# Scores of two steps in one bank, and z of the last tiles in halves, in a fused attention and expert kernel

## The chip, the cores and the metric
The kernel runs on one core of one Trainium2 chip. The metric is the device time of one execution in microseconds (us); lower is better. All times in this document are of that core. TensorE (PE) multiplies, VectorE (DVE), ScalarE (ACT) and GpSimd (POOL) work on its results, and SyncE (SP) issues the transfers. PSUM, into which PE writes, has eight banks of 512 fp32 columns on 128 partitions.

## The reference
For each of 4 batch entries ("rows" in the kernel) of 576 tokens:
```
scores = q k^T / 8 + bias(head) ; causal, window of 128 ; softmax ; @ v    (8 heads of 64)       stage 1
h = relu(x @ w_in) ; u, v = halves ; v = layernorm(v)
y = (u * (w_spatial @ v + b)) @ w_out                                                             stage 2
logits = y @ w_gate ; the two best of 4 experts, weights by softmax over the two
each expert e: q,k,v = y @ wq[e],wk[e],wv[e] (64 wide); full causal softmax(q k^T / 8) @ v @ wo[e]
out = sum over the chosen experts of weight * that                                                stage 3
```
All of it is in fp32 accuracy. Large products are made of three products of rounded parts (high by high, high by low, low by high), so almost every operand exists as a "high" part (ScalarE copies it out of PSUM) and a "low" part (VectorE subtracts the high part from the same PSUM bank).

## The kernel before
The order of the work on each engine is written out by hand, once per engine, and the engines meet at counting semaphores. The 576 tokens are five tiles, four of 128 and one of 64.

**Stage 1** of a row goes in 10 steps `m`, two steps to a tile of queries. A step holds two groups, `g = 2m` and `2m + 1`, of two heads each. The path of a group: PE `scores1(m)` (both groups of a step, L1199) writes banks 0 and 1; DVE `bias1(g)` (L833) adds the bias, writes the scores to a ring in SBUF and keeps the row minimum; ACT `exp1(g)` (L576); DVE `reciprocal1(g)` (L842, L844); POOL multiplies, `scale1(g)` (L471); PE `transpose1(g)` (L1242) into bank 2 or 3; ACT `copy_pt1(m)` (L617) copies the even group out and DVE `copy_pt1_second(m)` (L900) the odd one; PE `values1(g)` (L1280) multiplies by v. Every step's scores use the same two banks, so `scores1(m)` waits on `s1_bi` until the biases of step m - 1 have been added. `scores1` runs two steps ahead of the transposes (`AHEAD1 = 2`). In the first tile a head's scores are 128 columns wide, in the next three tiles 256, in the last 192. Step by step PE also does a piece of the product x @ w_in (`v_product`), from step 2 on (step 3 in row 0).

**Stage 3** first makes q and k of the experts in eight products `qk_product(0..7)` (L1212 to L1214). `high_qk(i)` on ACT (L709, L712) and `low_qk(i)` on DVE (L1103, L1108) take them out of PSUM. The products 4 to 7 reuse banks 2 and 3 in turn, so `qk_product(i)` waits until `low_qk(i - 2)` is done. Between them lie the scores of the first tiles (`scores3(w)`, L1429 and L1435, 18 units `w`). DVE also works out the weights of the experts, in two parts, `top2_a` and `top2_b` (`top2_b(0)` is L1042 to L1058, eight small operations one after the other). Then the loop of 8 steps: in a step PE does `transpose3` of two groups (L1447), the scores of two later units, an `out_product(b, i)` when z of tile i is ready (L1212 to L1214, L1218 and L1219 for the short tile), and `values3` of two groups (L1467). DVE `max3` (L1012), ACT `exp3` (L735), DVE `reciprocal3` (L1077, L1079), POOL `scale3` (L554), and the copies `copy_pt3` (ACT, L744) and `copy_pt3_second` (DVE, L1068) lie between. The tiles come in the order 0, 1, 4, 2, 3; tile i of this order ends in step 0, 1, 3, 5, 7. `values3` adds z transposed in bank 6 or 7 (by the parity of i); after a tile's last step `high_z(i)` (ACT, L749) and `low_z(i)` (DVE, L1084) take it out; `out_product` writes into the same bank; `copy_out(b, i)` (ACT, L608; for the short tile L604 and then `add_out`, DVE, L1091) takes the result out for the store.

**The seam.** While stage 3 of row b ends, stage 1 of row b + 1 begins: PE issues `scores1(b + 1, 0..2)` in the steps 5, 6 and 7, DVE and ACT interleave `bias1`, `exp1` and `reciprocal1` of the first groups, and `out_product(b, 4)` of the last tile comes in step 0 of the next row, behind its first two transposes. There are three such seams; the last row has none and ends with `out_product(3, 4)`, its copy and its store.

Of the kernel before, what the change touches and what calls it, by code (L numbers as in the profile page):

```python
# [27 lines left out]
P = 128  # L28
# [95 lines left out]
def build(nc, qT, kT, v, w_in, wsT, bsp, woT, wcat, wo, out):  # L124
    ctx = ExitStack()
    with ctx:
# [191 lines left out]
        def s1_banks(b, m):  # L318
            return (6, 7) if b == 0 and m == 1 else S1_BANKS

# [248 lines left out]
        def _(act):  # L569
# [40 lines left out]
            def row(b, first, more):  # L610
# [42 lines left out]
                for m in range(ND1):  # L653
                    if m % 2 == 0 and m >= 2:
                        high_x(m // 2 - 1)
                    if m == 0 and not first:
                        copy_pt1(0)
                        exp1(b, 3)
# [91 lines left out]

                if first:
# [69 lines left out]
        def _(dve):  # L821
            def bias1(b, g):
# [3 lines left out]
                at = w * (g % 2)  # L826
                dve.wait_ge(s1_sc, ND1 * b + g // 2 + 1)
                for n, (u, h) in enumerate(units1(g)):
                    if qb < NT - 1:
                        scores, table = bank[:, s1_banks(b, g // 2)[n], at:at + w], bias[:, h, c0:c0 + w]  # L830
                    else:
                        scores, table = bank[:, S1_BANKS[g % 2], 0:w], bias_last[:, h // 2, :]
# [60 lines left out]
            def row(b, first, more):  # L893
# [36 lines left out]
                for m in range(ND1):  # L930
                    if m % 2 == 0 and m >= 2:
                        low_x(m // 2 - 1)
                    if m == 1 or (m == 0 and not first):
                        copy_pt1_second(m)
                    if 2 * m + 4 < NG1:
# [3 lines left out]
                    if m > 1 or (m == 0 and first):  # L939
                        copy_pt1_second(m)  # L940
                    if 2 * m + 5 < NG1:
# [138 lines left out]

                def low_z(i):
                    dve.wait_ge(s3_zh, NT * b + i + 1)
# [57 lines left out]
                for m in range(ND3):  # L1140
                    for i in range(NT - 1):
                        if m == DEND3[i] + 1:
                            low_z(i)
                    if m and len(units3(m - 1)):
# [10 lines left out]
                    if m == DEND3[ORDER3.index(NT - 1)] + 2:  # L1155
                        add_out(ORDER3.index(NT - 1))
# [3 lines left out]
                    if more and m == ND3 - 3:  # L1160
                        bias1(b + 1, 0)
                        bias1(b + 1, 1)
                    if more and m == ND3 - 2:
# [16 lines left out]
        def _(pe):  # L1180
            def scores1(b, m):
# [7 lines left out]
                if m:  # L1189
                    if b or m != 1:  # L1190
                        pe.wait_ge(s1_bi, U1 * b + units1(2 * m if b or m > 2 else 2 * m - 2)[0][0])
                for j in range(2):
# [3 lines left out]
                    for odd in range(2):  # L1196
                        half = slice(D * odd, D * odd + D)
                        to = bank[:, s1_banks(b, m)[odd], w * j:w * j + w] if qb < NT - 1 else bank[half, S1_BANKS[j], 0:w]
# [46 lines left out]
            def out_product(b, i):  # L1245
                r = rows(ORDER3[i])
                pe.wait_ge(s3_zl, NT * b + i + 1)
                if i == 0 and b == 0:
                    pe.wait_ge(s_wlo, 2 * KT + NT + 2)
                for k in range(2):  # L1250
# [6 lines left out]
                last.then_inc(s3_om, 1)  # L1257
# [3 lines left out]
            def row(b, first, more):  # L1261
# [60 lines left out]
                for m in range(ND1):  # L1322
                    if (2 <= m or (m == 0 and first)) and m + AHEAD1 < ND1:
                        scores1(b, m + AHEAD1)
                    transpose1(b, 2 * m)
# [3 lines left out]
                    if m == 1:  # L1329
# [121 lines left out]
                def values3(g):  # L1451
# [6 lines left out]
                    elif es[0] == 0 and i >= 2:  # L1458
                        pe.wait_ge(s3_o, NT * b + i - 1)
                    if g % 2:  # L1460
# [3 lines left out]
                    for kb in ks:  # L1464
                        for j, e in enumerate(es):
                            c, at = place(qb, ks, len(es), j, kb), r * (e // 2)
                            last = nc.tensor.matmul(bank[D * (e % 2):D * (e % 2) + D, 6 + i % 2, at:at + r],  # L1467
# [27 lines left out]
                for m in range(ND3):  # L1495
# [8 lines left out]
                    for i in range(NT - 1):  # L1504
# [44 lines left out]
```

## Time and profile before
| | |
|---|---|
| median of 3 runs | 513.32 us (513.13 to 514.11) |
| the profiled execution | 514.02 us, span 512.2 us |
| PE busy | 493.8 us, 96% of the span |
| DVE, ACT, POOL busy | 300.5, 275.9, 201.3 us |
| TensorE clock granted | full in every slice |

The span is the time from the first to the last instruction. Busy time is summed over an engine's instructions; the chain of waits is followed back from the last instruction of the kernel to whatever released each step. A wait's idle time is counted from the modelled end of the matmul before it.

### The profile page before, as it was taken

Reading aid. Unit: us, or ns where it says so; the run is one execution under the profiler, and the core shown is the slowest. Engines: PE = TensorE matmul, PEld = TensorE weight load, DVE = VectorE, ACT = ScalarE, POOL = GpSimd, SP = SyncE. Lnnn points to the kernel's source line nnn. Section 1 sums busy time; section 2 is a strip of 40 time slices with the busy share of each in tenths; the row PEclk is TensorE's granted clock in tenths of the full one; section 3 lists DMA queues with packets and bytes.
Section 4 is the critical chain, followed back from the end, with each engine's and each line's share of the span. In section 5 each row is a group of like instructions: output and inputs, shape, how many; then the busy total and the mean of one; then the engine's idle time right before and its main releaser. Section 6 shows DMA issues by size and latency. Waiting matters only on the chain.

```text
span 512.2 us, 10892 instructions
## 1 busy us (share of the span) xinstructions
PE 493.8 (96%) x3981; PEld 426.5 (83%) x3981; DVE 300.5 (59%) x1116; ACT 275.9 (54%) x820; POOL 201.3 (39%) x376
## 2 busy tenths in 40 slices
PE   8899999999999999999998999999998999999996
PEld 5677998998767789999876789999876779999974
DVE  6976772567757743256757762237676664236671
ACT  6876472446567643255657743236557663234572
POOL 4765432212424633423424553341244455162240
PEclk9999999999999999999999999999999999999999
DMA  8909020023110070004110061002311000000111
GB/s 245 320 25 287 24 82 1 1 47 96 49 43 1 4 184 1 1 1 127 54 32 22 2 158 29 1 1 47 114 34 41 1 3 1 1 0 16 33 43 52
DMA packets 31785, 28.51 MB, mean 56 GB/s; under 512 B 5810, under 2 KB 24242, under 8 KB 31732
## 3 DMA queue, kind: packets, MB, share of 16 engines
q1 hardware_dynamic: 31732, 27.82, 18.4%
q8 instruction: 31, 0.51, 0.4%
q14 instruction: 22, 0.18, 0.1%
HBM read 20.74 MB, written 4.72 MB: 50 GB/s over the span
## 4 chain that ended last, share of the span: by engine, by line
PE 78%; DVE 12%; ACT 4%; issue 3%; POOL 1%; DVEq 0%; ACTq 0%
PE bank L1212 15%; PE bank L1213 14%; PE bank L1214 14%; PE bank L1199 7%; PE bank L1242 5%; PE bank L1280 5%; PE bank L1429 5%; PE bank L1467 4%; PE bank L1447 4%; DVE ring L833 2%; DVE neg L1012 2%; PE bank L1219 1%; PE bank L1218 1%; PE bank L1370 1%; PE bank L1372 1%
## 5 line engine op out<-in xcount | busy, mean ns | idle before, releaser
L471 POOL TENSOR_SCALAR ring<-ring,r 128x256 f32<-128x256 f32 (+2 forms) x144 | 68.2, 486 | 88.1 <-DVE r L844 87.8
L554 POOL TENSOR_SCALAR p<-p,r,wgt 128x128 f32<-128x128 f32 (+3 forms) x64 | 38.4, 613 | 91.3 <-DVE r L1079 64.5
L576 ACT ACTIVATE ring<-ring,neg 128x256 f32<-128x256 f32 (+2 forms) x144 | 67.8, 473 | 6.7 <-DVE neg L833 6.6
L735 ACT ACTIVATE p<-bank,neg 128x128 f32<-128x128 f32 (+4 forms) x72 | 39.1, 548 | 41.2 <-DVE neg L1012 41.1
L833 DVE CUSTOM_DVE_ANT_0 ring<-bank,bias 128x256 f32<-128x256 f32 (+1 forms) x128 | 43.8, 384 | 14.9 <-PE bank L1199 14.9
L1199 PE MATMUL bank<-k,q 64*128 64x256 f32 (+2 forms) x320 | 40.7, 375 | 4.4 <-DVE neg L833 4.4
L519 POOL TENSOR_TENSOR g_lo<-uT,g_hi 128x288 fp32r<-128x288 f32 x32 | 27.2, 873 | 42.6 <-ACT g_hi L697 42.6
L1280 PEld LDWEIGHTS bank<-pt,v_in 128*64 128x64 f32 x576 | 28.2, 136 | 14.8 <-issue 11.6
L1212 PE MATMUL bank<-g_hi,w_c_hi 128*128 128x288 f32 x128 | 38.5, 301 | 1.6 <-DVE k_lo L1108 1.6
L1280 PE MATMUL bank<-pt,v_in 128*64 128x128 f32 (+1 forms) x576 | 37.3, 268 | 1.5 <-ACT pt L617 1.4
L1242 PE MATMUL bank<-ident,ring 128*128 128x128 f32 (+1 forms) x256 | 37.6, 282 | 1.2 <-POOL ring L471 1.2
L1212 PE MATMUL bank<-w_spatial_hi,vn_hi 128*128 128x288 f32 x128 | 37.9, 296 | 0.5 <-DVE uT L997 0.5
L1212 PE MATMUL bank<-x_hi,w_in_hi 128*128 128x288 f32 x128 | 38.3, 300 | 0.0
L1012 DVE TENSOR_REDUCE neg<-bank 128x1 f32<-128x128 f32 (+4 forms) x72 | 33.9, 511 | 7.4 <-PE bank L1435 7.1
L1214 PE MATMUL bank<-x_hi,w_in_lo 128*128 128x288 f32 x128 | 37.8, 295 | 0.0
L1214 PE MATMUL bank<-g_hi,w_c_lo 128*128 128x288 f32 x128 | 37.8, 295 | 0.0
L1213 PE MATMUL bank<-g_lo,w_c_hi 128*128 128x288 f32 x128 | 37.8, 295 | 0.0
L1213 PE MATMUL bank<-w_spatial_lo,vn_hi 128*128 128x288 f32 x128 | 37.7, 295 | 0.0
L1214 PE MATMUL bank<-w_spatial_hi,vn_lo 128*128 128x288 f32 x128 | 37.7, 295 | 0.0
L1213 PE MATMUL bank<-x_lo,w_in_hi 128*128 128x288 f32 x128 | 37.7, 294 | 0.0
L1242 PEld LDWEIGHTS bank<-ident,ring 128*128 128x128 f32 (+1 forms) x256 | 26.9, 138 | 12.2 <-issue 8.0
L1199 PEld LDWEIGHTS bank<-k,q 64*128 64x128 f32 (+1 forms) x320 | 25.6, 182 | 13.3 <-issue 10.5
(182 smaller groups left out, 1387.6 us busy)
## 6 DMA issues: line engine op xcount, KB each, us to landing
v_in<-v SPq DMA_DIRECT2D x16, 256.0 KB, 4.7
out<-o_sb SPq DMA_DIRECT2D x16, 256.0 KB, 2.0
q<-qT SPq DMA_DIRECT2D x15, 256.0 KB, 4.6
k<-kT SPq DMA_DIRECT2D x15, 256.0 KB, 5.4
w_in_raw<-w_in SPq DMA_DIRECT2D x4, 512.0 KB, 6.2
w_cat_raw<-wcat SPq DMA_DIRECT2D x1, 1544.0 KB, 8.8
w_spatial_raw<-wsT SPq DMA_DIRECT2D x1, 1152.0 KB, 9.1
k_hi<-k_hi SPq DMA_DIRECT2D x8, 144.0 KB, 2.5
```

The costliest lines, as they stand in the source:

```text
L471: last = nc.gpsimd.tensor_scalar(p, p, r1[:, i % 2, h:h + 1], 0.0, ALU.mult, ALU.add)
L554: nc.gpsimd.tensor_scalar(p, p, r3[:, i % 2, e:e + 1], by, ALU.mult, ALU.mult).then_inc(s3_sd, 1)
L576: nc.scalar.activation(x, x, ACT.Exp, bias=neg1[:, u % SLOTS1:u % SLOTS1 + 1], scale=-1.0, accum_out=sum1[:, i % 2, h:h + 1]).then_inc(s1_ ...
L735: nc.scalar.activation(p3[:, w % P3_SLOTS, 0:n], scored3(w), ACT.Exp, bias=neg3[:, w % 4:w % 4 + 1], scale=1.0, accum_out=sum3[:, i % 2, e ...
L833: nc.vector.tensor_tensor_reduce(out=ring[:, u % SLOTS1, 0:w], in0=scores, in1=table, scale=-SCALE, scalar=3.0e38, op0=ALU.add, op1=ALU.mi ...
L1012: nc.vector.tensor_reduce(neg3[:, w % 4:w % 4 + 1], scored3(w), AX.X, ALU.max, negate=True).then_inc(s3_mx, 1)
L1199: last = nc.tensor.matmul(to, q1[half, k, tok(qb)], k1[half, k, k0:k0 + w], start=True, stop=True)
L1212: nc.tensor.matmul(to, hi_l, hi_r, start=first, stop=False)
L1213: nc.tensor.matmul(to, hi_l, lo_r, start=False, stop=False)
L1214: return nc.tensor.matmul(to, lo_l, hi_r, start=False, stop=last)
L1242: last = nc.tensor.transpose(bank[0:k, 2 + g % 2, c:c + P], ring[:, u % SLOTS1, P * j:P * j + k], ident[:])
L1280: last = nc.tensor.matmul(bank[D * (h % 2):D * (h % 2) + D, x_bank(i), at:at + r], v_in[:, kb, h, :], pt[:, g % 2, c:c + r], start=(kb == ...
```

## The change
Everything is a matter of order, of banks and of how finely a wait is cut; no product is added or left out.
- `together(b, m)`: the two steps of the first tile (rows 1 to 3) and of the last tile (all rows) write their scores side by side into the same two banks (4 x 128 and 2 x 192 columns). PE issues both steps in a run, the second without a wait; `bias1` waits for both.
- Seam, PE: `scores1(b + 1, 0)` and `(b + 1, 1)` both in step 5 of stage 3, nothing in step 6, `scores1(b + 1, 2)` in step 7 as before. In steps 1 and 2 of stage 1, `scores1(m + 2)` stands behind the transposes (before: in step 1 only, also in row 0). `scores1(9)` follows `scores1(8)` in step 6.
- Seam, ACT and DVE: `exp1` of the groups 0, 1, 2, 3 in the steps 5, 6, 7 and after the loop (before: 0, 1, 2 from step 6 on, 3 and 4 in step 0 of the next row); `bias1(4)` and `bias1(5)` and the reciprocals move forward in the same way.
- z of the last two tiles is taken out in two halves (k = 0 and 1, two experts each), each half in a bank of its own (`zt_bank`): the first half a step earlier, and `out_product` waits for each half by itself. In the last row `out_product(3)` is spread over the steps 6 and 7. `values3` of the second half waits until the `exp3` units have left banks 4 and 5.
- `copy_out(1)`, `copy_out(2)` and `copy_out(3)` on ACT come one step later, at the step's end.
- Start of stage 3: ACT does `high_qk(4)` between `exp3(1)` and `exp3(2)`; DVE does `reciprocal3(0)` and `low_qk(4)` ahead of `top2_b(0)`.

```diff
+        def zt_bank(i, k):
+            return {(NT - 2, 1): 5, (NT - 1, 1): 4}.get((i, k), 6 + i % 2)
+        def zt_half(i, k):
+            return bank[:, zt_bank(i, k), P * k:P * k + P]
+        def together(b, m):
+            return m >= ND1 - 2 or (b > 0 and m < 2)
...
ACT, start of stage 3
-                for w in range(4):
-                    exp3(w)
+                exp3(0)
+                exp3(1)
                 high_qk(4)
+                exp3(2)
+                exp3(3)
...
ACT, loop of stage 3
                 for m in range(ND3):
-                    for i in range(NT - 1):
+                    for i in range(NT - 2):
                         if m == DEND3[i] + 1:
                             high_z(i)
+                    for i in (NT - 2, NT - 1):
+                        if DEND3[i] <= m <= DEND3[i] + 1:
+                            high_z_half(i, m - DEND3[i])
                     copy_pt3(m)
                     for w in units3(m):
                         exp3(w)
-                    for i in range(NT - 1):
-                        if m == DEND3[i] + 1:
+                    if more and m >= ND3 - 3:
+                        exp1(b + 1, m - (ND3 - 3))
+                    if m == 1:
+                        copy_out(b, 0)
+                        exp_logits(1)
+                    for i in range(1, NT - 1):
+                        if m == DEND3[i] + 2:
                             copy_out(b, i)
-                    if m == 1:
-                        exp_logits(1)
-                    if more and m >= ND3 - 2:
-                        exp1(b + 1, m - (ND3 - 2))
-                high_z(NT - 1)
+                high_z_half(NT - 1, 1)
                 if more:
-                    exp1(b + 1, 2)
+                    exp1(b + 1, 3)
...
DVE, steps of stage 1
-                    if m == 1 or (m == 0 and not first):
+                    early = 1 <= m <= 2 or (m == 0 and not first)
+                    if m == 0 and not first:
+                        reciprocal1(b, 3)
+                    if early:
                         copy_pt1_second(m)
-                    if 2 * m + 4 < NG1:
+                    if 2 * m + 4 < NG1 and (m or first):
                         bias1(b, 2 * m + 4)
-                    if 2 * m + 3 < NG1:
+                    if 2 * m + 3 < NG1 and (m or first):
                         reciprocal1(b, 2 * m + 3)
...
DVE, start of stage 3
-                top2_b(0)
                 reciprocal3(0)
                 low_qk(4)
+                top2_b(0)
                 reciprocal3(1)
...
DVE, loop of stage 3
                     if more and m == ND3 - 2:
+                        reciprocal1(b + 1, 0)
                         bias1(b + 1, 2)
                         bias1(b + 1, 3)
-                        reciprocal1(b + 1, 0)
+                    if more and m == ND3 - 1:
+                        reciprocal1(b + 1, 1)
+                        bias1(b + 1, 4)
+                        reciprocal1(b + 1, 2)
+                low_z_half(NT - 1, 1)
                 if more:
-                    reciprocal1(b + 1, 1)
-                low_z(NT - 1)
-                if more:
-                    reciprocal1(b + 1, 2)
+                    bias1(b + 1, 5)
...
PE, steps of stage 1
-                    if (2 <= m or (m == 0 and first)) and m + AHEAD1 < ND1:
+                    if (3 <= m or (m == 0 and first)) and m + AHEAD1 < ND1 - 1:
                         scores1(b, m + AHEAD1)
+                        if m + AHEAD1 == ND1 - 2:
+                            scores1(b, ND1 - 1)
                     transpose1(b, 2 * m)
                     transpose1(b, 2 * m + 1)
                     if m == 0 and not first:
                         out_product(b - 1, NT - 1)
-                    if m == 1:
+                    if 1 <= m <= 2:
                         scores1(b, m + AHEAD1)
...
PE, loop of stage 3
-                    if more and m >= ND3 - 3:
-                        if m == ND3 - 3:
-                            pe.wait_ge(s3_ex, U3 * (b + 1))
-                        scores1(b + 1, m - (ND3 - 3))
-                    for i in range(NT - 1):
+                    if more and m == ND3 - 3:
+                        pe.wait_ge(s3_ex, U3 * (b + 1))
+                        scores1(b + 1, 0)
+                        scores1(b + 1, 1)
+                    if more and m == ND3 - 1:
+                        scores1(b + 1, 2)
+                    for i in range(NT - 2):
                         if m == DEND3[i] + 1:
                             out_product(b, i)
+                    if m == ND3 - 2:
+                        out_product(b, NT - 2, (0, 1) if more else (0,))
+                    if m == ND3 - 1 and not more:
+                        out_product(b, NT - 2, (1,))
```

## Rows read from the trace of the kernel before

**Rows 1.** The page: busy time by engine, and the chain that ended last.
```profile
PE 493.8 (96%) x3981; PEld 426.5 (83%) x3981; DVE 300.5 (59%) x1116; ACT 275.9 (54%) x820; POOL 201.3 (39%) x376
...
PE 78%; DVE 12%; ACT 4%; issue 3%; POOL 1%; DVEq 0%; ACTq 0%
```
**Rows 2.** Waits of PE: line, releaser: total us, times, longest us.
```profile
PE bank L1199 <- DVE neg L833: 4.4, 4, 1.3
PE bank L1467 <- ACT pt L744: 2.4, 5, 0.9
PE bank L1212 <- DVE zt L1084: 2.0, 4, 0.9
PE bank L1212 <- DVE k_lo L1108: 1.6, 4, 0.4
```
**Rows 3.** Timeline, PE, row 2, around `qk_product(6)`: start, length, instruction, [idle before].
```profile
351.45 0.22 PE L1435 MATMUL bank<-causalr,identr 128*128 128x128 f32 x1
352.07 0.40 PE L1212 MATMUL bank<-g_hi,w_c_hi 128*128 128x288 f32 x1 [0.40 <-DVE k_lo L1108]
```
**Rows 4.** The same stretch on DVE, then on ACT.
```profile
349.31 0.16 DVE L1042 TENSOR_SCALAR rank<-rank 128x12 f32<-128x12 f32 x1
...
351.11 0.90 DVE L1108 TENSOR_TENSOR k_lo<-bank,k_hi 64x288 fp32r<-64x288 f32 x2
...
352.34 0.92 DVE L1108 TENSOR_TENSOR k_lo<-bank,k_hi 64x288 fp32r<-64x288 f32 x2
...
350.22 1.65 ACT L712 CAST k_hi<-bank 64x288 fp32r<-64x288 f32 x4
```
**Rows 5.** Timeline, PE, steps 4 and 5 of stage 3 in row 2.
```profile
375.77 0.44 PE L1218 MATMUL bank<-w_o_hi,zt 128*128 128x512 f32 x1
...
378.45 0.71 PE L1199 MATMUL bank<-k,q 64*128 64x128 f32 x8
379.57 0.88 PE L1467 MATMUL bank<-pt,v_and_logits 128*64 128x128 f32 x12 [0.41 <-ACT pt L744]
```
**Rows 6.** The same steps on ACT, then on DVE.
```profile
375.04 0.26 ACT L749 CAST zt<-bank 128x128 fp32r<-128x128 f32 x1
...
378.33 0.58 ACT L604 COPY o_sb<-bank 64x512 f32<-64x512 f32 x1
...
375.34 0.29 DVE L1084 TENSOR_TENSOR zt<-bank,zt 128x128 fp32r<-128x128 f32 x1 [0.47 <-ACT zt L749]
```
**Rows 7.** Timeline, PE, the seam of rows 2 and 3: steps 0 to 2 of stage 1.
```profile
388.78 0.50 PE L1212 MATMUL bank<-w_o_hi,zt 128*128 128x512 f32 x1 [0.34 <-DVE zt L1084]
...
391.60 0.44 PE L1242 MATMUL bank<-ident,ring 128*128 128x128 f32 x2 [0.20 <-POOL ring L471]
391.97 1.13 PE L1199 MATMUL bank<-k,q 64*128 64x256 f32 x8
393.35 0.66 PE L1280 MATMUL bank<-pt,v_in 128*64 128x128 f32 x8 [0.25 <-ACT pt L617]
395.02 1.13 PE L1199 MATMUL bank<-k,q 64*128 64x256 f32 x8 [1.02 <-DVE neg L833]
396.09 1.09 PE L1242 MATMUL bank<-ident,ring 128*128 128x128 f32 x8
```
**Rows 8.** The same seam on DVE (reciprocal of group 5), then on POOL (groups 5, 6).
```profile
393.84 0.17 DVE L842 TENSOR_SCALAR den<-sum 128x2 f32<-128x2 f32 x1
...
394.30 1.89 POOL L471 TENSOR_SCALAR ring<-ring,r 128x256 f32<-128x256 f32 x4 [0.81 <-DVE r L844]
```
**Rows 9.** The end of the last row: PE, PE, then ACT.
```profile
499.58 0.88 PE L1467 MATMUL bank<-pt,v_and_logits 128*64 128x128 f32 x12 [0.91 <-ACT pt L744]
...
507.48 0.50 PE L1212 MATMUL bank<-w_o_hi,zt 128*128 128x512 f32 x1 [0.93 <-DVE zt L1084]
...
506.59 0.37 ACT L749 CAST zt<-bank 128x256 fp32r<-128x256 f32 x1 [1.30 <-PE bank L1467]
```
**Rows 10.** Row 0: PE at the second step of stage 1, and POOL later.
```profile
14.99 1.13 PE L1199 MATMUL bank<-k,q 64*128 64x256 f32 x8 [1.34 <-DVE neg L833]
...
18.93 1.95 POOL L471 TENSOR_SCALAR ring<-ring,r 128x256 f32<-128x256 f32 x2 [0.68 <-DVE r L844]
```

More of the change, by code:

```diff
@@ L657, in row @@
                         copy_pt1(0)
-                        exp1(b, 3)
+                        exp1(b, 4)
                         copy_out(b - 1, NT - 1)
@@ L749, in high_z, with high_z_half @@
                     nc.scalar.copy(zt[:, i % 2, :, zt_part(i, False)], zt_of(i)).then_inc(s3_zh, 1)
+                def high_z_half(i, k):
+                    act.wait_ge(s3_pv, NG3 * b + END3[i] - 1 + 2 * k)
+                    nc.scalar.copy(zt[:, i % 2, k, 0:P], zt_half(i, k)).then_inc(s3_zh, 1)
                 if first:
@@ L831, in bias1 @@
                     else:
-                        scores, table = bank[:, S1_BANKS[g % 2], 0:w], bias_last[:, h // 2, :]
+                        scores, table = bank[:, S1_BANKS[g % 2], w * (m % 2):w * (m % 2) + w], bias_last[:, h // 2, :]
                     nc.vector.tensor_tensor_reduce(out=ring[:, u % SLOTS1, 0:w], in0=scores, in1=table, scale=-SCALE,
@@ L932, in row @@
                         low_x(m // 2 - 1)
-                    if m == 1 or (m == 0 and not first):
+                    early = 1 <= m <= 2 or (m == 0 and not first)
+                    if m == 0 and not first:
+                        reciprocal1(b, 3)
+                    if early:
                         copy_pt1_second(m)
-                    if 2 * m + 4 < NG1:
+                    if 2 * m + 4 < NG1 and (m or first):
                         bias1(b, 2 * m + 4)
-                    if 2 * m + 3 < NG1:
+                    if 2 * m + 3 < NG1 and (m or first):
                         reciprocal1(b, 2 * m + 3)
-                    if m > 1 or (m == 0 and first):
+                    if not early:
                         copy_pt1_second(m)
-                    if 2 * m + 5 < NG1:
+                    if 2 * m + 5 < NG1 and (m or first):
                         bias1(b, 2 * m + 5)
@@ L1079, in reciprocal3, with low_z_half @@
                     nc.vector.reciprocal(r3[at], den3[at]).then_inc(s3_rc, 1)
+                def low_z_half(i, k):
+                    dve.wait_ge(s3_zh, z_count(b, i, k))
+                    at = zt[:, i % 2, k]
+                    nc.vector.tensor_tensor(at[:, P:2 * P], zt_half(i, k), at[:, 0:P].bitcast(F32), ALU.subtract
+                                            ).then_inc(s3_zl, 1)
                 def low_z(i):
[L1082 removed]
+                    dve.wait_ge(s3_zh, z_count(b, i, 0))
                     at = zt[:, i % 2]
@@ L1140, in row @@
                 for m in range(ND3):
-                    for i in range(NT - 1):
+                    for i in range(NT - 2):
                         if m == DEND3[i] + 1:
                             low_z(i)
+                    for i in (NT - 2, NT - 1):
+                        if DEND3[i] <= m <= DEND3[i] + 1:
+                            low_z_half(i, m - DEND3[i])
                     if m and len(units3(m - 1)):
@@ L1189, in scores1 @@
                 if m:
-                    if b or m != 1:
+                    if not (m % 2 and together(b, m)) and (b or m != 1):
                         pe.wait_ge(s1_bi, U1 * b + units1(2 * m if b or m > 2 else 2 * m - 2)[0][0])
@@ L1197, in scores1 @@
                         half = slice(D * odd, D * odd + D)
-                        to = bank[:, s1_banks(b, m)[odd], w * j:w * j + w] if qb < NT - 1 else bank[half, S1_BANKS[j], 0:w]
+                        if qb < NT - 1:
+                            c = w * (2 * (m % 2) * together(b, m) + j)
+                            to = bank[:, s1_banks(b, m)[odd], c:c + w]
+                        else:
+                            to = bank[half, S1_BANKS[j], w * (m % 2):w * (m % 2) + w]
                         last = nc.tensor.matmul(to, q1[half, k, tok(qb)], k1[half, k, k0:k0 + w], start=True, stop=True)
@@ L1243, in transpose1, with out_product @@
                 last.then_inc(s1_t, 1)
-            def out_product(b, i):
+            def out_product(b, i, ks=(0, 1)):
                 r = rows(ORDER3[i])
-                pe.wait_ge(s3_zl, NT * b + i + 1)
                 if i == 0 and b == 0:
                     pe.wait_ge(s_wlo, 2 * KT + NT + 2)
-                for k in range(2):
+                for k in ks:
+                    if k == ks[0] or i >= NT - 2:
+                        pe.wait_ge(s3_zl, z_count(b, i, k))
                     if r < P:
@@ L1256, in out_product @@
                                  wo_hi[:, k, :], wo_lo[:, k, :], k == 0, k == 1)
-                last.then_inc(s3_om, 1)
+                if ks[-1] == 1:
+                    last.then_inc(s3_om, 1)
             pe.wait_ge(s_tab, 1)
@@ L1459, in values3 @@
                         pe.wait_ge(s3_o, NT * b + i - 1)
+                    if i >= NT - 2 and es[0] == 2:
+                        pe.wait_ge(s3_ex, U3 * (b + 1) if i == NT - 1 else U3 * b + U3 - 2)
                     if g % 2:
@@ L1466, in values3 @@
                             c, at = place(qb, ks, len(es), j, kb), r * (e // 2)
-                            last = nc.tensor.matmul(bank[D * (e % 2):D * (e % 2) + D, 6 + i % 2, at:at + r],
+                            last = nc.tensor.matmul(bank[D * (e % 2):D * (e % 2) + D, zt_bank(i, e // 2), at:at + r],
                                                     v3[:, AT3[kb], D * e:D * e + D], pt[:, g % 2, c:c + r],
```

13 lines of the change are left out of this document (8 added, 5 removed).

## The prediction
> **What bounds the kernel now.** I read the page first: PE is busy 96% of the span and holds 78% of the chain that ended last [rows 1]. No matmul is added or dropped, so the change can only win PE's idle time, about 18 us, and part of that is start and end. The list of PE's waits says where: 4.4 us in front of `scores1`, 2.4 in front of `values3`, 2.0 in front of an `out_product`, 1.6 in front of a `qk_product` [rows 2]. The timeline then gives each its place, and the places repeat: each of the three seams has the same gaps to 0.01 or so, each row the same 0.40 at the start of stage 3, and the last row has its own end. So I work out one seam, one stage 3 and the end. The idle times shown are short by about 0.15: they count from a modelled end, and matmuls overlap. The first product after the scores would start at 351.52 (0.07 behind the short mask product at 351.45) and starts at 352.07: 0.55 to be won where 0.40 is shown [rows 3].
>
> The method is the same at every place: keep the issue order of each engine as the changed text has it, give every operation its length from the rows, and let it start at the latest of its engine's last operation and its releaser (plus 0.04: the cast ends at 375.30 and `low_z` starts at 375.34 [rows 6]).
>
> **Start of stage 3 (4 rows).** `qk_product(6)` waits for `low_qk(4)`, which stands behind `top2_b(0)`, from 349.31 to 350.82, and a reciprocal of 0.29 [rows 4]. After: ACT does `high_qk(4)` (a quarter of 1.65 per copy, two copies, 0.8) behind two of the four exponentials, from 349.5 to 350.35; `low_qk(4)` follows at 350.4 and ends at 351.3, before 351.52. So 0.55 to 0.6 is won. What is late next: `top2_b` (1.5) and a reciprocal now stand in front of `low_qk(5)`, which starts at about 353.05 instead of 352.34 [rows 4] and ends at 353.95; `qk_product(7)`, which had more than a microsecond to spare, now comes up at 353.75 and waits about 0.25. The delay runs on through two exponentials and `high_qk(6)` to `low_qk(7)`, for which the second transpose waits another 0.1. Net: -0.25 a row. GpSimd's first `scale3` starts 1.5 later, and has 4 us to spare.
>
> **Steps 3 to 6 of stage 3 (4 rows).** `copy_out(1)` moves from a free place on ACT to between `exp3(15)` and `high_z(2)`. There is no cover: `high_z(2)` starts at 375.04 right behind that exponential, `low_z(2)` ends at 375.63, and `out_product(2)` starts at 375.77 with some 0.08 to spare [rows 5, 6]. A full copy holds ACT for 0.49, so this product starts 0.41 to 0.44 later (0.3 in the last row, where DVE lacks a memset). That is a new wait in a place that has none. At least it costs 0.2 (if the overlap of copies is better than I take it), at most 0.5.
> In step 5 PE now loses 0.16 waiting for the last exponential and 0.47 in front of `values3(10)` (379.57, against 378.45 + 0.65), because `copy_out(2)` (378.33) stands ahead of the copy that it needs [rows 5, 6]. That copy moves behind, and the 0.65 of `scores1(1)`, drawn forward from step 6, covers the rest. What stays is the wait for the last exponential, which is itself later by the 0.44: about 0.3. So 0.6 is won, 0.3 is paid.
> In step 6 `out_product(3)`'s second half waits for z's second half, which ACT takes only after an exponential that itself waits for both steps' biases, and after `copy_out(2)`: about 0.1.
> Sum of a whole stage 3 with a seam: -0.25 + 0.44 - 0.62 + 0.32 + 0.12 = 0.0. The stage breaks even; what is won at its start is paid back at `out_product(2)`.
>
> **The halves of z.** One cast of 256 columns takes 0.37 [rows 9], one of 128 takes 0.26 [rows 6], so ACT pays 0.15 a tile and DVE as much, in steps where both idle. "VectorE: DVE Perf Modes" of the Trainium skill, section "The TRN2 errata", speaks against such cuts: a fixed cost per instruction, paid by every small tile. The trace agrees in kind. By that page's cycle figures an extra piece would be an estimated 0.14 on ACT; off the path it changes nothing.
>
> **The seam (3 of them).** From 388.2, where `out_product(4)` could start:
> - it starts at 388.78, waiting for the full `low_z` [rows 7]. After, the first half is long done, the second half (0.26 + 0.29) hides behind two transposes and three products: -0.4.
> - the fourth transpose waits 0.20 (0.36 with the overlap) for POOL [rows 7]. After, `exp1(3)` and `reciprocal1(3)` come before the copies of step 0, with 0.6 to spare: -0.36.
> - `scores1(3)` at 391.97 to the end of `scores1(4)` and both transposes of step 2 is now 396.09 + 0.85 = 396.94, so 4.97 [rows 7]. After: `scores1(3)`, `values1`, T4, T5, `scores1(4)`. But T5 needs group 5, and its reciprocal still stands behind `bias1(6)`, which waits for `scores1(3)`: that reciprocal comes at 393.84 and POOL starts at 394.30 [rows 8], 2.33 after `scores1(3)`; two units take half of 1.89, so T5 can start 3.33 after it, while PE is there after 1.06 + 0.58 + 0.51 = 2.15. **A new wait of about 1.15 in front of T5** takes the place of the 1.02 and the 0.25. Then 0.51 + 1.06: 4.90. Won: 0.1 by these rows, 0.3 by the chain of starts; I take 0.27.
> Sum: -1.03 a seam, -3.1 for three. Next to it `scores1(5)` has 0.7 to spare, `v_product` 0.9.
>
> **Row 0 and the last tile.** In row 0 the same swap at step 2 meets no `v_product`: `scores1(4)` (14.99, after 1.34 idle [rows 10]) starts 0.8 later, one pair of transposes is already done, but `scores1(5)` then waits for its bias. Between -0.2 and +0.2; I take +0.1. `scores1(9)` beside `scores1(8)`: PE has no gap in steps 6 to 9 of rows 1 to 3 and DVE still finds its scores in time (the biases wait 0.1 longer, behind 0.6 of slack): 0, and 0.3 at most if that slack is gone in one row.
>
> **The last row.** No seam fills PE here. V10's idle is 0.91 (1.13 with overlap) [rows 9]; without `copy_out(2)` ahead 0.86 stays: -0.27. `out_product(3)`'s second half (0.8) moves between the last transposes and `values3(14)`, and hides its copies: -0.35. At the end `out_product(4)` waits 0.93 at 507.48 for full high and low copies [rows 9]; after, its first three products (0.8) run while the half copies (0.26 + 0.29) do: -0.97. With -0.25 at the start and +0.3 at `out_product(2)`: -1.55.
>
> **Total:** -3.1 - 1.55 + 0.1 = -4.55 against the profiled execution (514.02, span 512.2, 1.8 around it, which stays). That execution lies 0.7 above the median of 513.32; the waits are the same in all, so I take the gain from the median: **508.8 us**.
>
> **The rivals.**
> (a) Parts of this do better: `copy_out(1)` finds room (4 x 0.4 less), or T5's wait is shorter than 1.15. Without the first 507.2; without the second 505.4. For it: each rests on a slack of a few hundredths. Against: both follow from program order and measured lengths.
> (b) The forward moves pay less: in each seam the ACT queue (exponential, `copy_out(2)`, second half of z, `copy_pt3(6)`) holds V12, which by my chain has only 0.2 to spare. If it comes 0.8 later, three seams give back 1.8 and 510.6 stands.
> (c) GpSimd is slowed on T5's chain. In row 0 two units of 0.94 in all took 1.95 while DVE subtracted one SBUF tile from another [rows 10]. Were T5's pair hit so, each seam would lose 1.0: 511.8. Against it: in the seam the same four units took 1.89 [rows 8], unhindered, beside the same biases, which read PSUM and one table. "SBUF — State Buffer" of the Trainium skill, section "Who interferes with whom", says a VectorE instruction with two SBUF inputs contends with a GpSimd read, one with a single SBUF input does not; by that rule, and by the trace, the forecast stands.
> (d) Slower than before: the ACT queue of (b), deeper. `exp1(b + 1, 0)` now stands in step 5, ahead of everything that V12 and the short tile's `add_out` need, and waits for DVE to take both steps' scores. I have it start at 380.4. If DVE's own queue (a wait for ACT's half of z, then the copy) starts that bias 2 us later, V12 moves by 1.8, and so does all behind it: 3 x 1.8 = 5.4, so 514.2. It decides from 1.7 us on. Against: DVE waits there 0.5 us for the scores, not the reverse.
>
> **How the numbers follow.** The forecast has 0.64 (507.6 to 510.2), (a) 0.12, (b) 0.10, (c) 0.05, no measurable change by several small losses 0.05, (d) 0.04. The range of 8 in 10 takes most of (a)'s first case and all of (b): 507.0 to 511.0. About 1 us (0.2%) is what a measurement can tell from no change; that makes 0.91 faster, 0.05 same, 0.04 slower.
>
> **What would show it.** Right: no wait at `qk_product(6)`, a small one at (7); a new wait of 0.3 to 0.4 `out_product` <- zt in step 4; none at `values3(10)` in a seam, 0.6 to 0.9 in the last row; `scores1` <- neg gone from the seams, and in its place L1242 <- ring of about 1 us, three times; 0.93 gone at the end. Wrong: V12 waiting for a copy, a wait of `scores1(2)` or (5), or T5 without a wait.

## The result, and the profile after

The changed kernel takes **509.71 us** (median of 4, 509.63 to 510.33) against 513.42 for the kernel before on the same chip (513.13 to 514.11): ratio **0.9924**, 95% interval 0.9909 to 0.994, so 3.7 us won. On a second chip it was 509.72 against 513.75, ratio 0.9917 (0.9902 to 0.9932). The forecast was 508.8, with a range of 507.0 to 511.0. The profiled execution took 509.63, with a span of 507.8: 4.4 less than the 512.2 of before, and again 1.8 around it. Of all executions in this document two are left out of the medians, both of experiment 4: 540.86 us, its profiled one, at a granted clock of 0.852, and 1193.14 us.

The page's busy times, to be held against [rows 1]:

```profile
PE 492.6 (97%) x3981; PEld 425.1 (84%) x3981; DVE 301.7 (59%) x1124; ACT 275.9 (54%) x828; POOL 200.4 (39%) x376
```

PE does the same 3981 matmuls in a span that is 4.4 shorter: 3.2 of that is idle time (18.4 before, 15.2 now), and 1.2 is busy time (493.8 before), to which the last section comes back. PE's waits after the change (line waiting, line waited for: total us, times, longest):

```profile
PE bank L1284 <- POOL ring L484: 4.7, 5, 1.0
...
PE bank L1254 <- DVE zt L1111: 0.9, 3, 0.3
PE bank L1241 <- DVE neg L857: 0.8, 1, 0.8
PE bank L1260 <- DVE zt L1117: 0.8, 3, 0.3
PE bank L1515 <- ACT pt L757: 0.6, 1, 0.6
```

Against [rows 2]: the 4.4 of `scores1` <- neg is down to 0.8, all in row 0; the 2.4 of `values3` <- pt to 0.6, in the last row; the 2.0 of `out_product` <- zt and the 1.6 of `qk_product` <- k_lo are gone. In their place stand a transpose of stage 1 waiting for GpSimd (1.2 us in the trace before, 4.7 now: 1.01 in each of the three seams and in row 0, and the 0.6 of before in row 0), and two small waits of `out_product` for z. (Lines have moved: L1241 is `scores1`, L1284 the transposes of stage 1, L1254 to L1256 the three products by the first copy of z and by others, L1475 `scores3`, L1493 the transposes of stage 3, L1515 `values3`.)

**The start of stage 3.** PE of row 2, to set beside [rows 3] (start, us, what, and in brackets the idle time shown before it):

```profile
349.44 0.22 PE L1481 MATMUL bank<-causalr,identr 128*128 128x128 f32 x1
349.50 0.35 PE L1254 MATMUL bank<-g_hi,w_c_hi 128*128 128x288 f32 x1
...
351.72 0.22 PE L1481 MATMUL bank<-causalr,identr 128*128 128x128 f32 x1
352.08 0.40 PE L1254 MATMUL bank<-g_hi,w_c_hi 128*128 128x288 f32 x1
...
356.68 0.97 PE L1493 MATMUL bank<-ident,p 128*128 128x128 f32 x4
357.40 0.48 PE L1475 MATMUL bank<-k_hi,q 128*128 128x512 f32 x1
```

`qk_product(6)` follows the mask product after 0.06, where it took 0.62 before. `qk_product(7)` follows after 0.36: a wait of about 0.3, which the list doesn't show. And the four transposes before the next scores last 0.97.

**Steps 4 to 6 of stage 3**, beside [rows 5]:

```profile
374.28 0.50 PE L1260 MATMUL bank<-w_o_hi,zt 128*128 128x512 f32 x1 [0.23 <-DVE zt L1117]
...
376.21 0.87 PE L1493 MATMUL bank<-ident,p 128*128 128x128 f32 x6
377.01 1.16 PE L1241 MATMUL bank<-k,q 64*128 64x128 f32 x16
378.11 0.88 PE L1515 MATMUL bank<-pt,v_and_logits 128*64 128x128 f32 x12
...
379.76 0.48 PE L1254 MATMUL bank<-w_o_hi,zt 128*128 128x512 f32 x1
...
381.01 0.51 PE L1254 MATMUL bank<-w_o_hi,zt 128*128 128x512 f32 x1 [0.30 <-DVE zt L1111]
```

The wait of `values3(10)` is gone; `out_product(2)` and the second half of `out_product(3)` each have a new one. The cause of the second stands on ACT and DVE:

```profile
379.46 0.58 ACT L617 COPY o_sb<-bank 64x512 f32<-64x512 f32 x1
380.07 0.27 ACT L766 CAST zt<-bank 128x128 fp32r<-128x128 f32 x1
```

```profile
380.08 0.68 DVE L1124 TENSOR_TENSOR o_sb<-bank,o_sb 64x512 f32<-64x512 f32 x1 [0.92 <-ACT o_sb L617]
380.69 0.27 DVE L1111 TENSOR_TENSOR zt<-bank,zt 128x128 fp32r<-128x128 f32 x1
```

The cast of z's second half stands behind the short tile's copy on ACT. On DVE the `add_out` of that copy (0.68) is ahead of the low half too.

**The seam**, beside [rows 7] and [rows 8], PE first, then DVE, then GpSimd:

```profile
386.05 0.66 PE L1284 MATMUL bank<-ident,ring 128*128 128x128 f32 x4
386.46 0.48 PE L1254 MATMUL bank<-w_o_hi,zt 128*128 128x512 f32 x1
...
388.61 0.66 PE L1284 MATMUL bank<-ident,ring 128*128 128x128 f32 x4
389.20 1.13 PE L1241 MATMUL bank<-k,q 64*128 64x256 f32 x8
...
390.85 0.66 PE L1284 MATMUL bank<-ident,ring 128*128 128x128 f32 x4
392.52 0.65 PE L1284 MATMUL bank<-ident,ring 128*128 128x128 f32 x4 [1.01 <-POOL ring L484]
393.11 1.13 PE L1241 MATMUL bank<-k,q 64*128 64x256 f32 x8
```

```profile
390.38 0.42 DVE L857 CUSTOM_DVE_ANT_0 ring<-bank,bias 128x256 f32<-128x256 f32 x1 [0.65 <-PE bank L1241]
...
390.73 0.42 DVE L857 CUSTOM_DVE_ANT_0 ring<-bank,bias 128x256 f32<-128x256 f32 x1
...
391.07 0.16 DVE L866 TENSOR_SCALAR den<-sum 128x2 f32<-128x2 f32 x1
```

```profile
391.53 1.89 POOL L484 TENSOR_SCALAR ring<-ring,r 128x256 f32<-128x256 f32 x4 [1.65 <-DVE r L868]
```

`out_product(4)` no longer waits: it starts 0.41 behind its four transposes, where it took 1.00 before. The forecast's new wait is there: the second four of the transposes (T5, those of group 5) start 3.32 after `scores1(3)`, after 1.01 of idle time shown. GpSimd waits for a reciprocal that DVE does at 391.07, behind two biases for which it first waited 0.65 for PE.

**The last row**, beside [rows 9]: `values3(10)` keeps its wait, `out_product(4)` at the end has none.

```profile
496.73 0.88 PE L1515 MATMUL bank<-pt,v_and_logits 128*64 128x128 f32 x12 [0.61 <-ACT pt L757]
...
503.05 0.50 PE L1254 MATMUL bank<-w_o_hi,zt 128*128 128x512 f32 x1
```

### The profile page after: what moved, and what is told of

Read it like the earlier page. It is cut to its first block, busy times and chain, and to the rows that moved or that the text cites. A ratio compares the mean times of both kernels' runs of the same rounds, so it can differ in the third digit from the quotient of the medians.

```text
span 507.8 us, 10924 instructions
## 1 busy us (share of the span) xinstructions
PE 492.6 (97%) x3981; PEld 425.1 (84%) x3981; DVE 301.7 (59%) x1124; ACT 275.9 (54%) x828; POOL 200.4 (39%) x376
## 4 chain that ended last, share of the span: by engine, by line
PE 74%; DVE 14%; ACT 5%; issue 3%; POOL 2%; DMA 1%; SPq 0%; DVEq 0%; ACTq 0%; POOLq 0%
PE bank L1254 14%; PE bank L1255 13%; PE bank L1256 13%; PE bank L1241 7%; PE bank L1284 6%; PE bank L1324 5%; PE bank L1515 4%; PE bank L1493 4%; PE bank L1475 4%; ACT p L748 2%; DVE neg L1039 2%; DVE k_lo L1141 1%; PE bank L1260 1%; DVE ring L857 1%; DVE q L1136 1%
## 5 line engine op out<-in xcount | busy, mean ns | idle before, releaser
L1284 PE MATMUL bank<-ident,ring 128*128 128x128 f32 (+1 forms) x256 | 37.8, 282 | 4.7 <-POOL ring L484 4.7
L1241 PE MATMUL bank<-k,q 64*128 64x256 f32 (+2 forms) x320 | 38.7, 369 | 1.2 <-DVE neg L857 0.8
L1284 PEld LDWEIGHTS bank<-ident,ring 128*128 128x128 f32 (+1 forms) x256 | 26.9, 138 | 14.8 <-POOL ring L484 7.7
L1254 PE MATMUL bank<-g_hi,w_c_hi 128*128 128x288 f32 x128 | 38.5, 301 | 0.6
L1254 PE MATMUL bank<-w_spatial_hi,vn_hi 128*128 128x288 f32 x128 | 37.9, 296 | 0.5 <-DVE uT L1024 0.5
L1254 PE MATMUL bank<-x_hi,w_in_hi 128*128 128x288 f32 x128 | 38.4, 300 | 0.0
L1256 PE MATMUL bank<-g_hi,w_c_lo 128*128 128x288 f32 x128 | 37.8, 295 | 0.0
L1256 PE MATMUL bank<-x_hi,w_in_lo 128*128 128x288 f32 x128 | 37.8, 295 | 0.0
L1256 PE MATMUL bank<-w_spatial_hi,vn_lo 128*128 128x288 f32 x128 | 37.7, 294 | 0.0
L710 ACT CAST g_hi<-uT 128x288 fp32r<-128x288 f32 x32 | 12.9, 433 | 38.3 <-DVE uT L1024 38.3
```

The lines of the kernel that those rows point to most:

```text
L1241: last = nc.tensor.matmul(to, q1[half, k, tok(qb)], k1[half, k, k0:k0 + w], start=True, stop=True)
L1254: nc.tensor.matmul(to, hi_l, hi_r, start=first, stop=False)
L1256: return nc.tensor.matmul(to, lo_l, hi_r, start=False, stop=last)
L1284: last = nc.tensor.transpose(bank[0:k, 2 + g % 2, c:c + P], ring[:, u % SLOTS1, P * j:P * j + k], ident[:])
```

## The experiments

**How they are read.** Medians of one kernel differed by little, single executions by more, and mostly at their beginning. The first `scores3` of row 0 began 105.32 into the span in the changed kernel's profile and 107.62 into that of the first experiment, which touches nothing ahead of it. The difference arises in the first 10 us, where PE waits for the inputs: the third run of `scores1` in row 0 starts at 8.14 in the one and at 10.12 in the other. From there on executions agree. So each experiment is also read by a sharper measure, the time from the first `scores3` of row 0 to that of row 3: three whole rows, three seams. The kernel before has 466.60 - 105.47 = 361.13, the changed one these two rows:

```profile
105.32 0.22 PE L1475 MATMUL bank<-k_hi,q 128*128 128x128 f32 x1
...
463.63 0.22 PE L1475 MATMUL bank<-k_hi,q 128*128 128x128 f32 x1
```

that is 358.31, and 358.25 on the second chip.

| kernel | median us (range) | ratio to before [95%] | three rows | per row against the changed kernel |
|---|---|---|---|---|
| before | 513.4 to 513.8 | | 361.13 | +0.94 |
| changed | 509.71 (509.63 to 510.33) | 0.9924 [0.9909, 0.994] | 358.31 | |
| changed, second chip | 509.72 (509.15 to 509.91) | 0.9917 [0.9902, 0.9932] | 358.25 | -0.02 |
| start order back | 509.36 (508.63 to 511.52) | 0.9916 [0.9897, 0.9936] | 358.01 | -0.10 |
| `copy_out(1)` back | 508.19 (507.58 to 508.5) | 0.9886 [0.9868, 0.9905] | 357.11 | -0.40 |
| reciprocal first | 506.63 (506.17 to 506.85) | 0.9857 [0.9836, 0.9878] | 355.38 | -0.98 |
| both halves waited | 513.99 (513.05 to 515.55) | 1.0001 [0.9989, 1.0013] | | |
| short tile's copy first | 507.95 (507.58 to 509.56) | 0.9889 [0.9871, 0.9906] | 356.50 | -0.60 |
| last tile apart | 510.40 (509.78 to 510.62) | 0.9931 [0.9915, 0.9946] | 358.85 | +0.18 |
| `top2_b` later | 506.66 (506.51 to 507.1) | 0.9862 [0.9843, 0.988] | 356.15 | -0.72 |
| four edits together | 499.25 (499.15 to 501.39) | 0.9722 [0.9709, 0.9736] | 350.09 | -2.74 |

**1. The start of stage 3 in the order of before.**

```
-                exp3(0)                    +                for w in range(4):
-                exp3(1)                    +                    exp3(w)
                 high_qk(4)                                  high_qk(4)
-                exp3(2)
-                exp3(3)
and on DVE top2_b(0) back ahead of low_qk(4)
```

> The changed kernel (509.7) with the old order at the start of stage 3 (ACT: the four exponentials, then high_qk(4); DVE: top2_b(0) ahead of reciprocal3(0) and low_qk(4)). Theory from the trace after: the new order wins 0.56 at qk_product(6) and loses it again at qk_product(7) and in front of the second transpose, so that the scores of unit 8 come 0.13 later than before, counted from the row's first scores. Then taking it back gives 0.1 a row: 509.2 (509.0 to 509.7). Rival, the step as forecast: the new order wins 0.25 a row, and without it the time is 510.7.

Measured: 0.10 a row less than the changed kernel, and in PE's waits the old wait is back:

```profile
PE bank L1252 <- DVE k_lo L1139: 1.6, 4, 0.4
```

So the changed kernel's order of the start removes four waits, 1.6 us in all as shown, and is no faster for it: 0.10 a row slower, where the forecast had 0.25 a row faster. (The two medians, 509.36 and 509.71, don't tell them apart; the three rows do.) The removed wait is paid in two smaller ones that the list doesn't show.

**2. `copy_out(1)` back to its place of before.**

```
-                        if m == DEND3[i] + 2:
+                        if m == DEND3[i] + (1 if i == 1 else 2):
```

> The changed kernel with copy_out(1) on ACT again in step 2 of stage 3's loop instead of step 3. Theory: this copy alone makes out_product(2) start 0.39 late in every row; the wait of L1260 on zt goes, and 4 x 0.39 = 1.5 with it: 508.2 (508.0 to 508.7). Rival: the wait hides others behind it (the last exponential, the second half of z), which then show: gain under 0.5, 509.3.

Measured: -0.40 a row, and the wait of `out_product(2)` has left the list. The term of +0.44 a row is the cost of that one copy's place. The list has a line that it lacked, the transposes at the start of stage 3 waiting for `low_qk(7)` (L1493 <- DVE q, 0.5 in three). It is no new wait: from these transposes to the next scores it is 0.72 in both kernels, and only the listing differs.

**3. In the seam, the reciprocal of group 5 ahead of the bias of group 6.**

```
+                    if m == 1:
+                        reciprocal1(b, 2 * m + 3)
                     bias1(b, 2 * m + 4)
-                    if 2 * m + 3 < NG1 and (m or first):
+                    if 2 * m + 3 < NG1 and (m > 1 or (m == 0 and first)):
```

> The changed kernel with reciprocal1(b, 5) ahead of bias1(b, 6) on DVE in step 1 of stage 1. Theory: T5's wait of 1.01 comes only from the reciprocal's place behind a bias that waits for scores1(3). Its exponential is done at 389.92 and PE is there at 391.4, so T5 no longer waits; scores1(4) then waits about 0.35 for bias1(7). Gain 0.86 in each of three seams and 0.6 in row 0: 506.5 (506.1 to 507.2). Rival: GpSimd or the exponential holds T5 anyway, gain at most 0.3 a seam: 508.8 or more.

Measured: -0.98 a row, 3 us in all. GpSimd's work is cut in two and T5 finds its input (PE, then GpSimd):

```profile
386.98 1.13 PE L1243 MATMUL bank<-k,q 64*128 64x256 f32 x8
...
389.77 1.13 PE L1243 MATMUL bank<-k,q 64*128 64x256 f32 x8
```

```profile
386.73 0.93 POOL L484 TENSOR_SCALAR ring<-ring,r 128x256 f32<-128x256 f32 x2 [0.42 <-DVE r L868]
388.20 0.94 POOL L484 TENSOR_SCALAR ring<-ring,r 128x256 f32<-128x256 f32 x2 [0.53 <-DVE r L868]
```

The two scores now start 2.79 apart, where the changed kernel has 3.91 (389.20 to 393.11). In row 0 the stretch from `scores1(3)` to the first `v_product` takes 8.13, where the changed kernel has 8.78. The new wait came from the order of DVE's queue alone: two instructions that wait for nothing stood behind one that waits for PE.

**4. `out_product` of the last two tiles waits for both halves of z.**

```
-                        pe.wait_ge(s3_zl, z_count(b, i, k))
+                        pe.wait_ge(s3_zl, z_count(b, i, 1 if i >= NT - 2 else k))
```

> The changed kernel in which out_product of the last two tiles waits for both halves of z before its first product; the halves are still copied separately. Theory: being able to start on the first half is worth 0.8 + 0.3 at out_product(3) and out_product(4) in each seam and 0.75 at the end, so 513.8 (513.0 to 514.3): as much as the whole change gains. Rival: only the end of the kernel needs it, since in the seams other waits take over: 510.5.

Measured: 513.99, the ratio to the kernel before is 1.0001. In its trace `out_product` waits for z in four places, `out_product(3)` in each seam and `out_product(4)` at the end of the last row. The other edits stay in it, and so does the cost of two small instructions for one large. So the early start on the first half is worth as much as the whole change: 4.3 us by the medians, which are of different chips, and about 4.0 by the two ratios. Without it, what the other edits win and lose comes to nothing together.

**5. The changed kernel again, on another chip**, as the base for what follows.

> The changed kernel, unedited, beside the three others: 509.7 on the first chip; 0.9924 of the time of before.

The times are in the table; the lists of waits are alike and three rows agree to 0.06 us.

**6. The short tile's copy ahead of the exponentials of the next row.**

```
+                    if m == DEND3[2] + 2:
+                        copy_out(b, 2)
                     ...
-                    for i in range(1, NT - 1):
+                    for i in (1, 3):
```

> The changed kernel with copy_out(2), the short tile's first half, ahead of exp1(b + 1, 0) on ACT in step 5. Theory: out_product(3)'s second half starts 0.45 late in each seam because this copy, and behind it z's second half on ACT and add_out on DVE, stand behind an exponential that waits for both steps' biases. Without that 3 x 0.45 = 1.35 is won: 508.4 (508.2 to 508.9). Rival: z's second half comes late by itself (values3(11) has to end first), gain under 0.3.

Measured: -0.60 a row. The wait of `out_product(3)`'s second half (L1254 <- zt, 0.9 in three) is gone from the list and that of `out_product(2)` remains (0.8 in three). The 0.30 shown a row was worth 0.60; by the starts it had cost 0.56 (see the last sections).

**7. The last tile's two steps of scores apart again.**

```
-            return m >= ND1 - 2 or (b > 0 and m < 2)
+            return b > 0 and m < 2
```

(and `scores1` of the last step back at its own turn.)

> The changed kernel with the last tile's scores of steps 8 and 9 issued apart again, as before (each in its own step and waiting for the biases of the step before). Theory from the trace: side by side the two runs take 1.45 instead of 0.80 + 0.79, and 0.19 in all is saved up to the next transposes though no wait was there; so 4 x 0.19 = 0.8 slower: 510.5 (510.2 to 510.8). Rival, the forecast: PE has no gap there, so no difference: 509.7.

Measured: +0.18 a row; the median is 0.7 above that of the changed kernel on that chip, where three to four rows of 0.18 make 0.5 to 0.7. Yet the lists of waits are the same but for a tenth, and PE has no gap in these steps in either. The rows of row 3, apart (first fence) and together (second):

```profile
410.11 1.09 PE L1324 MATMUL bank<-pt,v_in 128*64 128x128 f32 x16
411.13 0.87 PE L1241 MATMUL bank<-k,q 64*64 64x192 f32 x8
411.93 1.09 PE L1284 MATMUL bank<-ident,ring 128*128 128x128 f32 x8
...
415.45 0.87 PE L1241 MATMUL bank<-k,q 64*64 64x192 f32 x8
...
418.67 1.09 PE L1324 MATMUL bank<-pt,v_in 128*64 128x128 f32 x16
```

```profile
409.32 1.09 PE L1324 MATMUL bank<-pt,v_in 128*64 128x128 f32 x16
410.34 1.52 PE L1241 MATMUL bank<-k,q 64*64 64x192 f32 x16
411.79 1.09 PE L1284 MATMUL bank<-ident,ring 128*128 128x128 f32 x8
...
417.67 1.09 PE L1324 MATMUL bank<-pt,v_in 128*64 128x128 f32 x16
```

From the first values to the last it is 8.56 apart and 8.35 together. Apart, a run of 8 score matmuls takes 0.80 until the next begins (411.13 to 411.93); together, 16 take 1.45 (410.34 to 411.79), not 1.60.

**8. `top2_b(0)` behind the four small things that others wait for.** On DVE at the start of stage 3:

```
-                top2_b(0)
                 reciprocal3(1)
                 low_qk(5)
                 max3(4), max3(5)
+                top2_b(0)
```

> The changed kernel with top2_b(0) on DVE moved on, from behind low_qk(4) to behind max3(5), where DVE idles 1.5 us waiting for high_qk(6). Theory: the new order's 0.56 at qk_product(6) is lost again only because top2_b delays low_qk(5) and, through exp3 and high_qk(6), low_qk(7). Then both waits behind it go and 0.56 + 0.13 is won in each of four rows: 506.9 (506.6 to 507.6). Rival: GpSimd's scale3(0..3), which needs top2_b's weights and then starts 3 us later, becomes the wait in front of the first transposes: gain under 1.5 in all, 508.2 or more.

Measured: -0.72 a row, 3 us in all. Both unlisted waits are gone:

```profile
350.25 0.22 PE L1481 MATMUL bank<-causalr,identr 128*128 128x128 f32 x1
350.30 0.35 PE L1254 MATMUL bank<-g_hi,w_c_hi 128*128 128x288 f32 x1
...
354.84 0.60 PE L1493 MATMUL bank<-ident,p 128*128 128x128 f32 x4
355.20 0.48 PE L1475 MATMUL bank<-k_hi,q 128*128 128x512 f32 x1
```

`qk_product(7)` follows the mask after 0.05 and the transposes last 0.60. GpSimd, which needs what `top2_b` computes, has time: the one wait of PE for it in the list (0.2) is as long as before.

**9. The edits of 2, 3, 6 and 8 in one kernel.**

> The changed kernel with the four edits that each won: copy_out(1) in step 2, copy_out(2) ahead of the exponential, reciprocal1(b, 5) ahead of bias1(b, 6), top2_b(0) behind max3(5). If the four waits are independent their gains add: 1.5 + 1.7 + 3.1 + 3.0 = 9.3, 500.4. Rival: out_product(2)'s wait and the short tile's copy hide one another and the last exponential, so that a microsecond or two are shared: 501.5 to 502.5.

Measured: **499.25 us, ratio 0.9722 (0.9709 to 0.9736)**, faster than both kernels: 10.5 us below the changed one, 14.4 below the one before. A row is 2.74 shorter; the four edits alone gave 0.40 + 0.98 + 0.60 + 0.72 = 2.70. They add up, since each removes a wait of PE that the others don't touch. By the medians the gain, 10.5, is 1.0 more than the four gains together (1.5 + 3.1 + 1.8 + 3.1). The trace has 9.9: 8.22 in the three rows, 1.08 in the last row, 0.64 in the first steps of row 0; what the medians have beyond that lies in the beginning of the executions or in their spread, which wasn't separated. The four longest waits of PE that are left:

```profile
PE bank L1250 <- DVE pt_hi L873: 1.4, 1, 1.4
PE bank L1328 <- ACT pt L630: 1.2, 2, 0.9
PE bank L1288 <- POOL ring L484: 0.6, 1, 0.6
PE bank L1519 <- ACT pt L757: 0.5, 1, 0.5
```

None of these four recurs in every row, and PE is 98% busy.

## Why the prediction was right, and where it was off

**The method held.** Issue order, lengths from rows, and the latest of queue and releaser gave the places where PE waits, but for one that isn't there (the last exponential) and T5 in row 0, and the sign of what each part does to the time, but for the start of stage 3. In us of row 2, forecast against measured:

| part | forecast | measured |
|---|---|---|
| start of stage 3 | -0.25 | +0.13 (by experiment 1: +0.10) |
| `out_product(2)` waits for `copy_out(1)` | +0.44 | +0.44 (+0.39 to its start; experiment 2: 0.40) |
| `values3(10)`, with the 0.16 in front of `scores1(0)` | -0.62 | -0.47 |
| wait for the last exponential | +0.32 | 0.0 |
| second half of `out_product(3)` | +0.12 | +0.56 (+0.45 to its start) |
| `scores1(0)`, `(1)` side by side | 0 | -0.37 |
| seam: `out_product(4)` | -0.4 | -0.59 |
| seam: fourth transpose | -0.36 | -0.45 |
| seam: the swap with the new wait of T5 | -0.27 | 0.0 |
| the last tile's scores | 0 | -0.19 |
| a row | -1.03 | -0.94 |
| last row | -1.55 | -1.43 |

The measured terms are differences of starts in the two traces, rounded, and sum to -0.94; the row, read by itself, has the same. Three rows give 361.13 - 358.31 = 2.82, the last row 1.43, and 0.15 lies ahead of the first `scores3`: 4.40, the difference of the spans (512.2 - 507.8). Forecast: 4.55. Of what lies ahead, the swap in row 0 was forecast at +0.1; from `scores1(3)` to the first `v_product` it is 8.59 before and 8.78 after, +0.19, and T5 waits there too.

That the row came out within 0.09 is in good part luck. Four terms were too good, by 0.38, 0.15, 0.44 and 0.27, and five too bad, by 0.32, 0.37, 0.19, 0.09 and 0.19; the two sides cancel.

**Terms mis-sized.**
- *The start of stage 3.* The step "the second transpose waits another 0.1" for `low_qk(7)`: it waits about 0.37 (0.97 for four transposes instead of 0.60). The delay of `low_qk(5)` arrives whole: counted from the mask product ahead of `qk_product(6)`, that subtraction starts 0.78 later than before and `low_qk(7)` 0.77 later (5.94 behind the mask before, 6.71 after), while PE gets to the transposes earlier. The 0.55 won at `qk_product(6)` is thus less than the 0.3 and 0.37 paid behind it. Experiment 1 shows the sign, experiment 8 the cause: moving `top2_b` behind them gives 0.72.
- *The second half of `out_product(3)`.* The forecast's 0.12 left out that on ACT and on DVE the short tile's work stands ahead of the second half of z: a copy of 0.61 and an `add_out` of 0.61, one after the other. The product starts its second half 0.45 late, and from there to the next values it takes 0.1 more than before. Experiment 6 takes this away and wins 0.60 a row.
- *The swap in the seam.* By the rows it was worth 0.1, by the chain of starts 0.3; I took the better, and it was 0.0. T5 itself came 3.32 behind `scores1(3)`, for a forecast 3.33; behind it `scores1(4)` started after 0.59 where I took 0.51.
- *The last exponential.* The 0.16 in front of `scores1(0)` was read as a wait for it, and a later exponential was to make it 0.32. It is no such wait. `scores1(0)` starts 0.80 behind its six transposes before and after, and in experiment 9 too, where the exponential ends earlier (0.64 behind their start, 0.70 in the changed kernel). Eight transposes are followed by scores just as much later than by a product, 1.02 for 0.85, with no exponential to wait for.
- *The scores side by side*, here and in the last tile, were priced at nothing, and win 0.37 and 0.19. Of the 0.37, 0.20 is the run of scores (1.10 for 2 x 0.65) and 0.17 is that one change from transposes to scores is saved.

**From the row sum to the median.** I laid the gain of one profiled execution (514.02) on a median 0.7 below it. Against its own execution the forecast was 509.5, and the changed kernel's profiled execution took 509.63. The 0.9 us by which 508.8 missed is mostly this step. The "waits are the same in all", but the beginning isn't: the first `scores3` of row 0 lies between 104.9 and 107.6 in kernels that are alike up to there. The profiled execution of the kernel before, with 105.47, isn't a late one. Which of its others began earlier I can't say, since only one was profiled here, so the 0.7 has no cause shown.

**The rivals.** (b), the values of group 12 (V12) held by ACT's queue: no wait there. (c), GpSimd slowed on T5's chain: the four units took 1.89 as before, beside two biases again. The rule of the Trainium skill weighed in the forecast ("SBUF — State Buffer", section "Who interferes with whom") thus agrees once more. (d), DVE 2 us late with the first biases of the next row: no, they start at 378.22, after 0.24 of waiting for the scores, and `exp1(b + 1, 0)` at 378.56. (a), that parts do better: neither half of it came by itself, but experiments 2 and 3 are its two halves made true by an edit, 0.40 and 0.98 a row, and (a) had priced them at 0.4 a row (four rows) and at 3.4 us for three seams (3 measured).

**What carried the gain** was not seen in the forecast as clearly as the runs show it: with both halves waited for, nothing of the gain is left (experiment 4). It had -0.4 a seam, and -0.35 and -0.97 in the last row, for the halves: 2.5 us. Experiment 4 says 4.0 to 4.3: without the early start `out_product(3)` waits in the seams too, which the forecast had not counted for the halves.

## What to carry to other kernels

Look in each in-order queue for an instruction that waits, with others behind it that could go: two moves of this kind on VectorE (a reciprocal ahead of a bias, a weight computation behind the subtractions) won 3 us each, nearly as much as the whole change (3.7). A matmul that needs two pieces, with the first piece handed over by itself, hides the copy of the second behind its own first products. And after such a change follow each delay to the end of its chain: a wait taken off PE's list was paid back in two places where the list shows nothing.

## What the runs showed of the hardware that was not expected

**Like matmuls in one run cost less.** The scores read 64 rows, what stands around them 128. Two runs of eight next to each other took 1.45 in place of 1.60, and the stretch of experiment 7 was 0.21 shorter, with the same matmuls and no wait shown; the wider ones, `scores1(0)` and `(1)` in step 5, run in 1.10 for 2 x 0.65. Behind transposes, `scores1` starts 0.17 to 0.18 later than a product or `scores3` does: after four transposes 0.59 (388.61 to 389.20) against 0.41 (386.05 to 386.46), and in both traces after six 0.80 against 0.63, after eight 1.02 against 0.85. Behind 16 matmuls of values nothing of the kind shows: 1.02 to 1.03, to scores and to transposes alike. So that the change between 64 and 128 rows costs it, and not the change of line, bank or kind of matmul, isn't shown, and wasn't tried.

**Idle time on PE is shown too small.** 0.30 shown was 0.45 lost by the start of the product, 0.56 by that of the values behind it, and 0.60 by experiment 6; 0.3 of `qk_product(7)` and 0.37 in a group of four transposes aren't shown at all. The Trainium skill says why this can be ("Perfetto Trace Analysis", section "Tensor Engine Instruction (MATMUL, LD_WEIGHTS)"): the end of a matmul in the profile is estimated, not observed. The traces agree: eight transposes at 411.79 that are shown to end 1.09 later are followed at 412.64. Differences of starts are what to go by.
